# Loading q, k and v of an attention stage in two arrays of 256 KB in place of one of 512 KB

## What is computed

```python
for b in range(nb):
    qb, kb, vb = (q[:, :, sl], k[:, :, sl], v[:, :, sl])
    intra = np.einsum('bhic,bhjc->bhij', qb, kb) * Dmask[None]
    intra = np.einsum('bhij,bhjd->bhid', intra, vb)
    inter = np.einsum('bhid,bhde->bhie', qb * lam_pow[None], kv_state)
    out[:, :, sl] = intra + inter
    kb_dec = kb * rev_pow[None]
    kv_state = lam_block[None, :, None, None] * kv_state + np.einsum('bhsd,bhse->bhde', kb_dec, vb)
...
k = np.maximum(xk @ w_k, 0.0)
v = k * k @ w_v
r = 1.0 / (1.0 + np.exp(-(xr @ w_r)))
return (r * v).astype(np.float32)
...
return (gate * val @ w_out).astype(np.float32)
```

## Time and profile before

| | us |
|---|---|
| three runs, median | 277.01 |
| lowest and highest of them | 276.48 and 277.29 |
| the profiled execution, its own time | 276.0 |
| its span (first to last instruction) | 274.2 |
| PE busy | 269.9 (98%) |
| DVE, ACT, POOL busy | 166.0, 125.4, 23.6 |
| DMA | 22.57 MB in 7506 packets |

### The profile page before, as it was taken

How to read it: one execution, slowest core, us unless ns; L and a number is a source line. 1 busy time by engine, 2 the same in 40 slices (tenths; PEclk the granted TensorE clock), 3 DMA queues, 4 the chain that set the end, 5 groups by cost and what they waited for, 6 DMA issues and landing times.

```text
span 274.2 us, 4270 instructions
## 1 busy us (share of the span) xinstructions
PE 269.9 (98%) x1746; PEld 226.3 (83%) x1746; DVE 166.0 (61%) x258; ACT 125.4 (46%) x223; POOL 23.6 (9%) x25
## 2 busy tenths in 40 slices
PE   8999999999999999999999999999999999999996
PEld 7889977888888888888888888888888888888886
DVE  5866999998581125465885553429969599325000
ACT  2237788977582124365721234748217306412121
POOL 1667750000000000000000000000000000000000
PEclk9999999999999999999999999999999999999999
DMA  7999996000000000000000000530000000310323
GB/s 215 408 410 406 406 407 253 0 0 2 0 0 0 2 0 0 0 2 0 0 0 2 2 0 0 174 134 0 0 0 2 0 0 0 117 38 0 115 82 111
DMA packets 7506, 22.57 MB, mean 82 GB/s; under 512 B 960, under 2 KB 1216, under 8 KB 7488
## 3 DMA queue, kind: packets, MB, share of 16 engines
q1 hardware_dynamic: 7488, 22.31, 21.4%
HBM read 19.16 MB, written 3.15 MB: 81 GB/s over the span
## 4 chain that ended last, share of the span: by engine, by line
PE 96%; DVE 2%; DMA 1%; issue 0%; ACT 0%
PE ps L717 28%; PE ps L719 28%; PE ps L718 28%; PE ps L799 4%; PE ps L733 4%; PE ps L783 2%; PE ps L761 2%; DMA prm<-in_prm 1%; DVE dec L608 1%; DVE pT L508 0%; DVE qdec L589 0%; ACT out_sb L414 0%
## 5 line engine op out<-in xcount | busy, mean ns | idle before, releaser
L717 PE MATMUL ps<-xk_h,wk_h 128*128 128x512 f32 x96 | 37.5, 391 | 0.0
L718 PE MATMUL ps<-xk_l,wk_h 128*128 128x512 f32 x96 | 37.4, 389 | 0.0
L719 PE MATMUL ps<-xk_h,wk_l 128*128 128x512 f32 x96 | 37.4, 389 | 0.0
L717 PE MATMUL ps<-kk_h,wv_h 128*128 128x512 f32 x96 | 37.3, 389 | 0.0
L718 PE MATMUL ps<-kk_l,wv_h 128*128 128x512 f32 x96 | 37.3, 389 | 0.0
L719 PE MATMUL ps<-kk_h,wv_l 128*128 128x512 f32 x96 | 37.3, 389 | 0.0
L571 DVE SCALAR_TENSOR_TENSOR gate<-x,prm,gate 128x512 f32<-128x512 f32 x48 | 32.6, 748 | 0.0
L547 DVE SCALAR_TENSOR_TENSOR kk_f<-ps,ring 128x512 f32<-128x512 f32 x24 | 16.6, 691 | 24.1 <-ACT ring L367 24.1
L384 ACT ACTIVATE gate<-x,prm 128x512 f32<-128x512 f32 x12 | 8.7, 725 | 43.2 <-DVE x L557 43.2
L367 ACT ACTIVATE ring<-ps 128x512 f32<-128x512 f32 x24 | 14.3, 597 | 26.7 <-PE ps L719 26.7
L717 PEld LDWEIGHTS ps<-xk_h,wk_h 128*128 128x128 f32 x96 | 18.0, 188 | 4.0 <-issue 0.3
(11 more groups left out here) (74 smaller groups left out, 487.5 us busy)
## 6 DMA issues: line engine op xcount, KB each, us to landing
qk<-in_qk SPq DMA_DIRECT2D x12, 512.0 KB, 11.3
kv<-in_kv SPq DMA_DIRECT2D x9, 512.0 KB, 12.8
out<-out_sb SPq DMA_DIRECT2D x11, 256.0 KB, 2.0
wk_raw<-in_w_k SPq DMA_DIRECT2D x4, 512.0 KB, 14.2
wv_raw<-in_w_v SPq DMA_DIRECT2D x4, 512.0 KB, 12.5
wr_raw<-in_w_r SPq DMA_DIRECT2D x2, 512.0 KB, 15.0
w_raw<-in_w_val SPq DMA_DIRECT2D x2, 512.0 KB, 4.4
w_raw<-in_w_out SPq DMA_DIRECT2D x2, 512.0 KB, 6.9
```

The lines of the kernel that those rows point to most:

```text
L717: nc.tensor.matmul(to, left(0), right(0), start=(i == 0), stop=False)
L718: nc.tensor.matmul(to, left(0), right(1), start=False, stop=False)
L719: done = nc.tensor.matmul(to, left(1), right(0), start=False, stop=(i == last))
```

## The change

From chunk 3 on (`WHOLE = 3`) q and k come from an array `q_k_in` in which all of a chunk's q lies ahead of all of its k, as two transfers of 256 KB with rows of 2 KB that follow each other without gaps. k and v come in the same way from `k_v_in`; of chunks 5 and 11 only v is loaded, now from an array without gaps. Chunks 0 to 2 are loaded as before. Both transfers of a load add 16 to the same semaphore, and two functions count what has to be there:

```diff
+WHOLE = 3
...
+        def qk_signals(n):
+
+            return 16 * sum(1 if m < WHOLE else 2 for m in range(n % IN_BUFS, n + 1, IN_BUFS))
+
+        def kv_signals(n):
+
+            return 16 * sum(1 if m < WHOLE or not has_update(m) else 2 for m in range(n % IN_BUFS, n + 1, IN_BUFS))
...
             def load_qk(n):
                 free(n)
-                sp.dma_start(qk[n % IN_BUFS][:, :, :], qk_in[n]).then_inc(qk_here[n % IN_BUFS], 16)
+                here = qk_here[n % IN_BUFS]
+                if n < WHOLE:
+                    sp.dma_start(qk[n % IN_BUFS][:, :, :], qk_in[n]).then_inc(here, 16)
+                else:
+                    for z in range(2):
+                        sp.dma_start(qk[n % IN_BUFS][:, z, :], q_k_in[n - WHOLE, z]).then_inc(here, 16)
 
             def load_kv(n):
                 free(n)
-                first = 0 if has_update(n) else 1
-                sp.dma_start(kv[n % IN_BUFS][:, first:, :], kv_in[n, :, first:, :]).then_inc(kv_here[n % IN_BUFS], 16)
+                here = kv_here[n % IN_BUFS]
+                if n < WHOLE:
+                    sp.dma_start(kv[n % IN_BUFS][:, :, :], kv_in[n]).then_inc(here, 16)
+                else:
+                    for z in range(0 if has_update(n) else 1, 2):
+                        sp.dma_start(kv[n % IN_BUFS][:, z, :], k_v_in[n - WHOLE, z]).then_inc(here, 16)
...
-                pe.wait_ge(qk_here[i], 16 * (n // IN_BUFS + 1))
+                pe.wait_ge(qk_here[i], qk_signals(n))
...
-        "qk": np.stack([features(q), features(k)], axis=2),
+        "qk": np.stack([features(q), features(k)], axis=2)[:WHOLE],
         "v0": tokens(v)[0],
-        "kv": np.stack([tokens(k[:, order]), tokens(v)], axis=2),
+        "kv": np.stack([tokens(k[:, order]), tokens(v)], axis=2)[:WHOLE],
+        "q_k": np.stack([features(q), features(k)], axis=1)[WHOLE:],
+        "k_v": np.stack([tokens(k[:, order]), tokens(v)], axis=1)[WHOLE:],
```

More of the change, by code:

```diff
@@ L50, in out_half, with build @@
     return row ^ (a >= PAIRS // 2)
-def build(nc, prm_in, qk_in, v0_in, kv_in, w_k, w_v, w_r, w_val, w_out, out):
+def build(nc, prm_in, qk_in, v0_in, kv_in, q_k_in, k_v_in, w_k, w_v, w_r, w_val, w_out, out):
     with ExitStack() as ctx:
@@ L282, in decay_k @@
                     i = n % IN_BUFS
-                    pool.wait_ge(kv_here[i], 16 * (n // IN_BUFS + 1))
+                    pool.wait_ge(kv_here[i], kv_signals(n))
                     if n >= 4:
@@ L294, in decay_q @@
                     i = n % IN_BUFS
-                    pool.wait_ge(qk_here[i], 16 * (n // IN_BUFS + 1))
+                    pool.wait_ge(qk_here[i], qk_signals(n))
                     if inters(n - 4 if n >= 4 else 0) > 0:
@@ L750, in update @@
                 i = n % IN_BUFS
-                pe.wait_ge(kv_here[i], 16 * (n // IN_BUFS + 1))
+                pe.wait_ge(kv_here[i], kv_signals(n))
                 if n == 0:
```

## The result

| | us |
|---|---|
| before, median of 22 runs (lowest and highest) | 276.63 (275.70 to 277.32) |
| with the change, median of 22 runs | 277.22 (276.64 to 278.91) |
| ratio, 95% interval | 1.0027 (1.0016 to 1.0039) |
| the profiled execution after, and its span | 277.23, 275.4 |

The change costs 0.27%, or 0.75 us (0.44 to 1.08) of 276.63; the medians alone differ by 0.59 us, the means by 0.76. That is on the edge of the 0.3% that I called no change, inside the range, and to the slower side; I had forecast 0.04 us. The loss is mostly at the lower end: 7 of the 22 executions before took 275.94 us or less, none with the change took less than 276.64. At the upper end, 277.32 stands against 277.55, with two of 278.22 and 278.91 beyond it.

The account below looks back on a forecast made before the run. TensorE's chain was taken to set the pace, with loads hidden by small slacks; issue cost nothing and slower rows exposed 0.04 us at chunk 5, so 277.01 became 277.05, forecast as 277.1 us, range 276.2 to 278.2.

Parts of the forecast that it names:

- Movement: DMA queue: 2 KB rows in place of 4 KB make each split load 0.07 us slower, bounds 0 and 0.09.
- Issue: SP's queue: sixteen more issues, 6.9 us, hidden and costed at nothing; SP's lead shrinks to about 7 us at worst.
- The rate that I gave for 15 to 33 us: Sign in the DMA queue that the forecast is right: 395 to 408 GB/s between 15 and 33 us.
- Chunk 5's q and k are the 4th split: 0.28 us late, 0.24 covered: At scores(5) on TensorE: four splits of 0.07 us against 0.24 us of slack leave 0.04 us exposed.
- k and v of chunk 3: 0.21 against 0.9: GpSimd's work for inter(3): the 3rd split lands 0.21 us late against 0.9 us of slack, so no cost.
- behind that VectorE has its own queue: At w_k's first piece: 1.05 us late against 1.1 us of slack, nothing exposed, with VectorE's own queue behind it.
- The signs: Trace after: about 9810 packets, w_k's first piece at 34 to 35 us, no new TensorE gap over 0.2 us.
- The third rival: TensorE's 0.61 us stop in attend(8) goes as smaller rows let something pass sooner: 276.4 us; chance 0.10.
- The first rival: Small rows cost more once most traffic is small; shows from d = 0.155 us a split, 279.3 at 0.25; chance 0.12.
- the second: Rival: each DMA transfer has its own price whatever its size, 2.7 us a split, giving 316 us; chance 0.01.

Follow-up runs that it names:

- the first run: Changed kernel's new arrays with 2 KB rows, but each load from chunk 3 on one 512 KB transfer; 1.0012 (0.9997 to 1.0027) against the kernel before.
- run 3: Changed kernel with WHOLE = 8, so only chunks 8 to 11 come in halves; 1.0020 (1.0008 to 1.0031) against the kernel before.
- run 9: Run 6 with VectorE's fourth mix of x put right behind the other three; 1.0016 (1.0000 to 1.0032) against the kernel before.
- run 5: Kernel before, but GpSimd waits before kdec(6) for k and v of chunk 7; 1.0036 (1.0020 to 1.0052) against the kernel before.
- run 7: Changed kernel with the load of v of chunk 5 moved behind k and v of chunk 7; 1.0022 (1.0009 to 1.0036) against the kernel before.
- run 10: Run 7 with VectorE's fourth mix of x put right behind the other three; 1.0016 (0.9996 to 1.0036) against the kernel before.
- run 11: Run 7 with the fourth mix early and k of chunk 3 loaded ahead, on its own wait; 1.0005 (0.9988 to 1.0022) against the kernel before.
- run 8: Run 6 with k of chunk 3 on its own semaphore, then q and k of 5, then v of 3; 0.9987 (0.9972 to 1.0002) against the kernel before.
- run 12: Run 8 with VectorE's fourth mix of x put right behind the other three; 0.9989 (0.9972 to 1.0006) against the kernel before.
- run 6: Kernel before with the load of v of chunk 5 moved behind k and v of chunk 7; 0.9996 (0.9979 to 1.0014) against the kernel before.

## Why the prediction was right, and where it was not

The range held the time, and 0.27% is inside what I called no change, if at its edge. But 0.75 us are not 0.04: the answer came out right from a sum with wrong parts, and that it did so was in part luck.

- **Movement** was right in kind and size. A split costs 0.076 us where I took 0.07, and the first run shows that the rows do it. The estimate from "DMA: Bandwidth & Descriptors" of the Trainium skill, section "Why small descriptors are slow (HBM only)", was 0.03 us; the measurement decides, and that is too low for this kernel. The rate that I gave for 15 to 33 us, 395 to 408 GB/s, was too high, since I had thinned the 4% out over loads that are not split; it is 388.
- **Issue** was rightly costed at nothing, but the lead of "about 7 us" was too low: the second half of q and k of chunk 8 is issued at 16.43 and lands at 26.84, 10.4 us later. SP comes to q and k of chunk 8 at 15.90 where it was 9.98, as halves shrink its lead, and the DMA engines don't run dry.
- **"Chunk 5's q and k are the 4th split: 0.28 us late, 0.24 covered"** failed in the 0.24. It was read from an execution with a late start (scores(2) at 9.82; 9.06 in the trace after). In the trace after, scores(5) waits 0.58 us, and from there on TensorE has nothing left to cover a later landing: scores(6) and (7) wait too. How much of those 0.58 us the kernel before has on average is not known, since only the one execution of it was profiled; runs 3 and 9, with whole loads to that point and early starts, have 0.5 and 0.7.
- **"k and v of chunk 3: 0.21 against 0.9", and the later ones with it, "nothing"** is the step that failed most. I asked whether GpSimd's result comes in time for TensorE, and it does. I did not ask what GpSimd's work lies beside when it is later. Nor did I follow VectorE: "behind that VectorE has its own queue" was true, and that queue had no slack at all: wk_l is ready at 40.51 and the matmul starts at 40.65, and after, when it certainly waits for wk_l, it starts by the same 0.15 us later (41.75 and 41.90). So VectorE set this moment before the change too, though the chain of waits named TensorE. In the traces the queue's 1.24 us are the difference between before and after; run 5 shows that GpSimd's place alone can make such a loss. How much of that place is owed to the halves is not shown (0.7 us of GpSimd's lateness came in one step, and run 3 has such steps with whole loads).
- The signs: w_k's first piece at 34 to 35 us (it is used at 34.87, with a wait of 0.3), the packets, and no new gap over 0.2 us before (wrong: 0.58), w_k's first matmul at 40.7 to 40.9 (wrong: 41.90). GpSimd's waits for k and v grew by 2.0 us in all (6.3 to 8.3) where I had said 1, and they did not cost nothing. The third rival didn't come: the stop in attend(8) is 0.56 us. Its premise, something that comes through the same full engines, has the packets of the instruction queue on its side; only smaller rows don't let them pass sooner, 1.1 us for one before and after.
- The first rival (rows far dearer, d = 0.155 and up) and the second (a price for each transfer) are refuted by 0.076 and by the first run.

What stays open: how the 0.75 us are shared between TensorE's waits for data and VectorE's chain. The profiled execution before was a quick one (276.0 against a median of 276.63) and the one after was at its median, so the 1.25 us between the traces are more than the change costs, and runs 7, 10 and 11, which ease one or both, differ by less than their intervals. Open too is what the stop in scores(9) does to the comparison. Neither the trace before nor the one after has it. Of the traces with whole loads (but for k and v of chunk 3 in runs 8 and 12) and nothing late on purpose, runs 8 and 9 have it and took 277.21 and 277.02 us; the one before and runs 6 and 12 don't, and took 276.00, 276.00 and 275.82. If it comes and goes in the kernel before in the same way, it makes the two ends of that kernel's range, and the change, in whose trace VectorE holds TensorE up to 41.90 anyway, loses mostly against the short executions. Nothing shows it for executions that weren't profiled.

## What to carry to other kernels

When loads come later, look not only at who waits for them but at what the work that they start will lie beside: a VectorE instruction with two inputs in SBUF that starts under one of GpSimd's was through only 0.55 us after that one here, at more than twice its time in the worst cases (1.76 us for 0.74). A slack of a few tenths that is read from one execution is worth no more than the start of that execution; compare how the chain and the loads start before one uses the difference. An engine whose queue runs without a pause up to a hand-over is at its limit even if the chain of waits names another. To split a transfer into rows of 2 KB costs about 6% of the rate here even with memory laid out for it, and gained nothing here, where everybody waits for both halves.

## What the runs showed of the hardware

- Rows of 2 KB move at 386 to 387 GB/s and rows of 4 KB at 409, in a queue that is full either way; the number of transfers and of semaphore writes made no difference that the rate shows.
- Transfers of 256 KB into 64 partitions in rows of 4 KB move at 228 GB/s.
- A mix of 128x512 with both inputs in SBUF takes 0.69 us alone (2.07 for three in run 8) and 1.53 on average with GpSimd busy beside it all the time (4.59 for three in run 5). Where a GpSimd instruction ends beside it, it ends 0.55 us after that one (61 of 61 mixes and differences), and GpSimd's qd goes from 1.27 to 1.72 us.
- A packet of 16 KB of the instruction queue takes 1.1 us of one DMA engine beside full loads, and TensorE's stops in attend(8) and scores(9) end 2.3 to 2.6 us after such a packet starts.
- The first small transfer, of 20 KB, was in use between 2.38 and 3.59 us in executions that issue it in the same way.
